# Attention heads on TensorE: the matmuls of a step put in another order

## Chip, cores and metric

One core of a Trainium2 chip runs the whole program. The metric is the time of one execution in microseconds (us). Engines are called as the profile calls them: PE is TensorE (PEld its weight loads), DVE is VectorE, ACT is ScalarE, POOL is GpSimd, SP is the queue that issues most DMAs.

## What is computed

Causal attention with a second term from a memory, for 4 x 8 = 32 heads of S = 576 rows and D = 64 columns, and behind it two MLP layers on 2304 tokens. The change touches the heads alone.

```python
scores = scale * q @ k.T                 # causal: -1e9 above the diagonal
a = exp(scores - scores.max(-1)); a /= a.sum(-1) + 1e-9
local = a @ v
q_p = where(q > 0, q, exp(q) - 1) + 1
mem_out = (q_p @ M_prev) / (q_p @ z_prev + 1e-6)
x = g * mem_out + (1 - g) * local        # g = sigmoid(beta) of the head
h = relu(x @ w_in); y = (s * h*h + b) @ w_out       # first MLP, d_ff 2048
# second MLP: softmax-gated unit, layer norm, product with the second w_out
```

## The kernel before

**Stages.** The program computes all heads, then the first MLP in five chunks of tokens, then the second MLP. In the profiled execution the regular part of the heads lies between about 50 and 226 us of the span, their end between 226 and 256 us, and the MLPs behind it.

**Two kinds of matmul.** Products of queries and keys are split in a high and a low part and run as fp32r; each is one matmul instruction. Everything else of a head is fp32: the product of weights and values and the memory product run as two instructions for each matmul call, and a transposition (a "turn") is one instruction. Each instruction has its own weight load in front of it.

**What PE does for head h.** `rows_of_scores(h, t)` (line 565) computes the scores of row tile t, only so that DVE can find the maximum of each row (`row_maximum`, line 967, written to `least`). The five tiles come in three groups: `first_rows` (tiles 4 and 1), `second_rows` (3), `third_rows` (0 and 2). All share two banks of PSUM, `ps_s`: tile 3 overwrites tile 4, and tiles 0 and 2 overwrite tile 1 and the turned maxima. So `second_rows` waits for DVE's maximum of tile 4, `third_rows` for that of tile 1 and for the copy of the turned maxima. The maxima of the head before are turned in the same group (line 594), copied by DVE (`negT`, line 976) and spread by POOL into `Q1` (line 394). Two steps later `cross(h, c)` (lines 631 and 632) computes the transposed scores of chunk c = 0 to 3, with the maxima already taken off by the second matmul of each block, into one of the two banks of `ps_x` (c mod 2); ACT takes the exponential (`exp_weights`, line 786, into `pT`), and POOL masks the diagonal tiles (line 406). One step after that `weigh_values(h, ts)` (line 650) multiplies `pT` with the values for the row tiles ts: tile t takes t + 1 calls, so two instructions times 1, 2, 3, 4, 5. The weights of tile 4 are 64 columns wide, those of the others 128, and so are those of one block of `cross(h, 0)` (64) and all other blocks (128).

**A step.** `steps` of `tensor` runs step h from 4 on: `first_rows(h+2)`, the crosses of head h, `weigh_values` of head h-1, `second_rows` and `third_rows` of head h+2, and work of pairs of heads. With pr = h // 2, an even step has `turn_output(pr-2)` and `turn_keys(pr+3)`, an odd step `turn_queries(pr+3)` and `memory(pr+1)`. A turn is five transpositions (line 486), memory is ten instructions (line 556). The last keys are turned in step 24, the last queries in step 25, the last rows of scores in step 29.

**What lies beside it.** Each engine works through its own program in order; semaphores are the only ties.
- DVE in step h: `first_rows` (copy of `negT`, two maxima), `second_rows`, `third_rows`; then in an even step `cut_keys(pr+3)` (line 1032, two instructions, after ACT's `round_keys`) and `scale_local(pr-1)` (lines 1057 to 1065), which divides the values product of a pair and frees the bank `ps_v` of the next pair's: `weigh_values` of an even head waits for it. In an odd step `scale_memory(pr+1)`.
- ACT: the four exponentials, and between them `copy_output`, `copy_queries`, `repeat_queries`, `feature_relu`, `feature_exp`, `round_keys` (line 818).
- POOL: masks, the spread of the maxima, rounding and cutting of the queries, `add_halves` (line 413), which makes the pair's output that `turn_output` turns; behind head 31 the cutting of the first MLP's weights (lines 1218 to 1229), for which PE's first MLP matmuls (line 1256) wait.
- SP: loads, and `stack`, which puts high and low halves one above the other after ACT's and POOL's cuts.

Of the kernel before, what the change touches and what calls it, by code (L numbers as in the profile page):

```python
# [12 lines left out]
P = 128  # L13
# [8 lines left out]
def need(eng, sem, value):  # L22

    if not isinstance(value, int) or value > 0:
        eng.wait_ge(sem, value)
# [84 lines left out]
def attention(nc, whole, ctx, xT, xq, ident, q, k, v, M_prev, z_prev, beta):  # L110
# [50 lines left out]
    least = [sb(f"least{s}", [P, P]) for s in range(2)]  # L161
# [50 lines left out]
    def is_pair(p):  # L212
        return 0 <= p < NPAIR

    def is_head(h):
        return 0 <= h < HEADS
# [264 lines left out]
    def tensor(pe):  # L481
# [24 lines left out]
        def turn_keys(p):  # L506
            pe.wait_ge(k_in[p % 2], 16 * Q_DMAS * (p // 2 + 1))
            if p == 0:
                pe.wait_ge(cleared_dve, PSUM_CLEARS)
            elif p == 1:  # L510
                act_placed(pe, 0, "k_own0")
                pe.wait_ge(k_lo_done, 1)
            else:
                pe.wait_ge(qT_copied, max(p, 3) if p != 3 else 4)
                need(pe, t_mem_done, p - 2)
                need(pe, xT_done, p - 4)
            turn(pair_tiles(first_k[p] if p < DIRECT else k_raw[p % 2]), kT_turned, keys_psum(p))
# [51 lines left out]
        def first_rows(h):  # L569
            if h == 0:  # L570
                pe.wait_ge(cleared, FOR_ROWS)
            if h < 2 * DIRECT:
                p = h // 2
                if h == 0:
                    act_placed(pe, 0, "q_hi1")
                    dve_placed(pe, 0, "q_lo0")
                elif h == 1:
                    act_placed(pe, 0, "q_hi1")
                    dve_placed(pe, 0, "q_lo1")
                elif h == 2:  # L580
                    act_placed(pe, 1, "q_cut0")
                    dve_placed(pe, 1, "q_lo0")
                else:
                    act_placed(pe, 1, "q_own1")
                    dve_placed(pe, 1, "q_lo1")
            elif h < HEADS:
                p = h // 2
                pe.wait_ge(stack_landed[p % SLOTS][h % 2], 16 * STACK_DMAS * stacks_sent(p))
            need(pe, maxed, 4 * min(h, HEADS))
            if h < HEADS:  # L590
                rows_of_scores(h, 4)
                ins = rows_of_scores(h, 1)
            if is_head(h - 1):
                ins = pe.transpose(ps_s[:, NEG_AT:NEG_AT + P], least[(h - 1) % 2][:, :], ident[:, :])
            ins.then_inc(scored, 1)

        def second_rows(h):
# [9 lines left out]
        def cross(h, c):  # L607
            a, p, par = slot(h), h // 2, h % 2
            kept = KEPT[par]
            if h == 0 and c == 0:  # L610
                pe.wait_ge(k_lo_done, 1)
                act_placed(pe, 1, "q_hi1")
                dve_placed(pe, 1, "q_lo0")
                pe.wait_ge(cleared, FOR_FIRST)
                pe.wait_ge(cleared_dve, DVE_CLEARS + 1)
            if h == 2 and c == 0:
                pe.wait_ge(cleared, POOL_CLEARS)
            if c == 0:
                pe.wait_ge(neg_spread, h + 1)
                if p < DIRECT:  # L620
                    pe.wait_ge(repeated, p + 1)
                    act_placed(pe, p, "q_own1")
                    pe.wait_ge(k_lo_done, p + 1)
                else:
                    pe.wait_ge(q_again, p - DIRECT + 1)
            need(pe, exped, h * NC + c - 1)
            at = 0
            for j, lo, hi in CHUNKS[c]:
                some = slice(P * j, P * j + rows_of[j])
                out = ps_x[0:rows_of[j], c % 2, at:at + hi - lo]  # L630
                pe.matmul(out, stacked[:, a, 1, some], stacked[:, a, 0, lo:hi], start=True, stop=False)  # L631
                ins = pe.matmul(out, K1[0:kept, p % LATE, par, some], Q1[0:kept, p % SLOTS, par, lo:hi],  # L632
                                start=False, stop=True)
                at += hi - lo
            ins.then_inc(crossed, 1)

        def weigh_values(h, ts):
            par = h % 2
            if 0 in ts:
                p = h // 2  # L640
                pe.wait_ge(tri_done, (h + 1) * NT)
                pe.wait_ge(v_in[p % 3], 16 * Q_DMAS * (p // 3 + 1))
                need(pe, t_loc_done, p)
                if h < 2:
                    act_placed(pe, 1, "k_own1")
                    pe.wait_ge(k_lo_done, 2)
            for t in ts:
                for j in range(t + 1):
                    at, m = p_at[j] + P * (t - j), rows_of[t]
                    ins = pe.matmul(ps_v[0:m, par, E1 * t:E1 * (t + 1)], pT[par][:, at:at + m],  # L650
                                    v_raw[h // 2 % 3][:, j, par, :], start=(t == 0),
                                    stop=(j == t), skip_group_check=True)
            if NT - 1 in ts:
                ins.then_inc(pv_done, 1)

        def steps(hs):
            for h in hs:
                pr, even = h // 2, h % 2 == 0
                ahead, here, behind = is_head(h + 2), is_head(h), is_head(h - 1)
                if ahead or is_head(h + 1):  # L660
                    first_rows(h + 2)
                if here:
                    cross(h, 0)
                if even and is_pair(pr - 2):
                    turn_output(pr - 2)
                if not even and is_pair(pr + 3):
                    turn_queries(pr + 3)
                if behind:
                    weigh_values(h - 1, (0, 1))
                if ahead:  # L670
                    second_rows(h + 2)
                if here:
                    cross(h, 1)
                if behind:
                    weigh_values(h - 1, (2,))
                if even and is_pair(pr + 3):
                    turn_keys(pr + 3)
                if ahead:
                    third_rows(h + 2)
                if here:  # L680
                    cross(h, 2)
                if behind:
                    weigh_values(h - 1, (3,))
                if here:
                    cross(h, 3)
                if not even and is_pair(pr + 1) and pr + 1 > 0:
                    memory(pr + 1)
                if behind:
                    weigh_values(h - 1, (4,))

        warm_up()
        turn_keys(0)
# [80 lines left out]
    def scalar(act):  # L773
# [8 lines left out]
        def exp_weights(h, c):  # L782
            act.wait_ge(crossed, h * NC + c + 1)
            if c == 0:
                need(act, pv_done, h - 1)
            act.activation(pT[h % 2][:, chunk_at[c]:chunk_at[c] + chunk_width[c]],  # L786
                           ps_x[:, c % 2, 0:chunk_width[c]], ACT.Exp, scale=SCALE).then_inc(exped, 1)
# [104 lines left out]
        def steps(hs, aside=None):  # L892
            for h in hs:
                pr, even = h // 2, h % 2 == 0
                here = is_head(h)
                if here:
                    exp_weights(h, 0)
                    if aside:
                        aside(0)
                if even and is_pair(pr - 2):  # L900
                    copy_output(pr - 2)
                if not even and is_pair(pr + 3):
                    copy_queries(pr + 3)
                if here:
                    exp_weights(h, 1)
                    if aside:
                        aside(1)
                if is_pair(pr + 2):
                    if even:
                        repeat_queries(pr + 2, 0)  # L910
                    else:
                        feature_relu(pr + 2)
                if even and is_pair(pr + 3):
                    round_keys(pr + 3)
                if here:
                    exp_weights(h, 2)
                    if aside:
                        aside(2)
                if is_pair(pr + 2):
                    if even:  # L920
                        repeat_queries(pr + 2, 1)
                    else:
                        feature_exp(pr + 2)
                if here:
                    exp_weights(h, 3)
                    if aside:
                        aside(3)

        def let_go():
            act.wait_ge(maxed, 4 * HEADS)  # L930
# [1219 lines left out]
```

## Time and profile before

| | |
|---|---|
| Median of 3 runs | 856.83 us (856.77 to 857.05) |
| The profiled execution's own time | 856.63 us |
| Its span in the profile | 854.5 us |
| PE busy | 842.5 us (99%) |
| DVE, ACT, POOL busy | 514.5, 340.6, 341.5 us (60%, 40%, 40%) |
| Granted TensorE clock | 9 in tenths in each of the 40 slices, 1.00 in the windows |
| Matmuls of the values, line 650 | 960, mean 254 ns |
| Rows of scores, line 565 | 192, mean 370 ns |
| Transposed scores, line 631 | 192, mean 320 ns |

How to read it: a matmul's record is longer than the time it takes of PE, because the next one starts before it has ended (960 matmuls of line 650 with a mean of 254 ns have 107.6 us of busy time between them). So what a matmul costs is read from the distance of starts, not from lengths. The record of a matmul and that of its weight load are two lines of the trace.

### The profile page before, as it was taken

The page shows a single profiled execution, that of the slowest core. Times are in us where ns is not written, and L with a number is a line of the kernel's source. Part 1 is how long each engine was busy: PE and PEld are TensorE (multiplying, and loading weights), DVE is VectorE, ACT ScalarE, POOL GpSimd, SP SyncE. Part 2 cuts the span into 40 slices and gives each one's busy share as a digit, 9 for nine tenths or more (in the row PEclk, how much of TensorE's full clock was granted, in tenths as well). Part 3 has the DMA queues.
Part 4 walks back from the last instruction along what each step waited for, and adds up shares of the span by engine and source line. Part 5 has one row for each costly group of instructions (what it writes and reads, how often), then busy time and mean ns, then how long its engine had stood idle before and what let it go on. Part 6 is the DMA issues. An engine that isn't in the chain of part 4 may idle for free.

```text
span 854.5 us, 13137 instructions
## 1 busy us (share of the span) xinstructions
PE 842.5 (99%) x4912; PEld 745.8 (87%) x4912; DVE 514.5 (60%) x1052; ACT 340.6 (40%) x607; POOL 341.5 (40%) x452
## 2 busy tenths in 40 slices
PE   8999999999999999999999999999999999999998
PEld 7899999999888888888888889999999888888886
DVE  7766657666547865433443334335767997777763
ACT  6665555565442223222322222224335534444422
POOL 5665656565659994000000000000648853334400
PEclk9999999999999999999999999999999999999999
DMA  8665666656403332000000000000101200000001
GB/s 147 141 150 131 149 144 135 149 129 132 119 5 106 107 105 75 1 0 1 1 1 0 1 1 1 1 1 1 30 21 49 62 26 25 26 25 17 21 25 49
DMA packets 86365, 49.35 MB, mean 58 GB/s; under 512 B 65056, under 2 KB 73248, under 8 KB 86304
## 3 DMA queue, kind: packets, MB, share of 16 engines
q1 hardware_dynamic: 83760, 47.94, 23.3%
q10 hardware_dynamic: 2544, 0.59, 0.4%
q8 instruction: 39, 0.64, 0.3%
q14 instruction: 22, 0.18, 0.1%
HBM read 27.28 MB, written 4.72 MB: 37 GB/s over the span
## 4 chain that ended last, share of the span: by engine, by line
PE 90%; DVE 7%; issue 2%; POOL 1%; ACT 0%; POOLq 0%; ACTq 0%
PE ps_h L1256 8%; PE ps_y L1273 8%; PE ps_h L1258 8%; PE ps_y L1272 8%; PE ps_h L1257 8%; PE ps_y L1271 8%; PE ps_v L650 7%; PE ps_s L565 4%; PE ps_r L1725 4%; PE ps_r L1724 4%; PE ps_r L1723 4%; PE ps_hid L1660 3%; PE ps_hid L1658 3%; PE ps_hid L1659 3%; DVE spent L967 3%
## 5 line engine op out<-in xcount | busy, mean ns | idle before, releaser
L1373 DVE TENSOR_TENSOR xT<-xT 128x512 f32<-128x512 f32 (+1 forms) x80 | 61.7, 772 | 125.6 <-ACT xT L1331 125.5
L1273 PE MATMUL ps_y<-g_hi,wout 128*128 128x512 f32 (+1 forms) x320 | 117.5, 367 | 0.0
L1272 PE MATMUL ps_y<-g_lo,wout 128*128 128x512 f32 (+1 forms) x320 | 117.5, 367 | 0.0
L1271 PE MATMUL ps_y<-g_hi,wout 128*128 128x512 f32 (+1 forms) x320 | 117.4, 367 | 0.0
L1557 POOL TENSOR_TENSOR win<-stage,win 128x512 fp32r<-128x512 f32 x2 | 2.6, 1294 | 281.8 <-ACT win L1792 281.8
L650 PE MATMUL ps_v<-v_raw,pT 128*128 128x65 f32 (+1 forms) x960 | 107.6, 254 | 1.2 <-DVE t_loc L1065 1.2
L650 PEld LDWEIGHTS ps_v<-v_raw,pT 128*128 128x128 f32 (+1 forms) x960 | 101.3, 173 | 6.9 <-issue 4.7
L967 DVE CUSTOM_DVE_ANT_0 spent<-ps_s,mask 128x576 f32<-128x576 f32 (+4 forms) x160 | 81.6, 539 | 42.4 <-PE ps_s L565 41.6
L1256 PE MATMUL ps_h<-x_hi,win 128*128 128x512 f32 (+1 forms) x280 | 103.0, 368 | 0.0
L1258 PE MATMUL ps_h<-x_hi,win 128*128 128x512 f32 (+1 forms) x280 | 102.8, 367 | 0.0
L1257 PE MATMUL ps_h<-x_lo,win 128*128 128x512 f32 (+1 forms) x280 | 102.8, 367 | 0.0
L1337 ACT ACTIVATE g_hi<-xT 128x512 fp32r<-128x512 f32 (+1 forms) x80 | 47.2, 590 | 137.2 <-DVE xT L1375 137.2
L786 ACT ACTIVATE pT<-ps_x 128x512 f32<-128x512 f32 (+3 forms) x128 | 64.2, 502 | 94.4 <-PE ps_x L632 93.5
L1331 ACT ACTIVATE xT<-ps_h 128x512 f32<-128x512 f32 (+1 forms) x80 | 44.2, 553 | 138.0 <-PE ps_h L1258 136.2
L1378 DVE TENSOR_TENSOR g_lo<-xT,g_hi 128x512 fp32r<-128x512 f32 (+1 forms) x80 | 65.8, 823 | 52.5 <-ACT g_hi L1337 52.5
L406 POOL TENSOR_SCALAR_AFFINE_SELECT pT<-pT 128x128 f32<-128x128 f32 (+1 forms) x160 | 42.7, 287 | 86.4 <-ACT pT L786 86.1
L1271 PEld LDWEIGHTS ps_y<-g_hi,wout 128*128 128x128 f32 x320 | 60.1, 188 | 7.6
L1273 PEld LDWEIGHTS ps_y<-g_hi,wout 128*128 128x128 f32 x320 | 60.1, 188 | 7.5
L1272 PEld LDWEIGHTS ps_y<-g_lo,wout 128*128 128x128 f32 x320 | 60.1, 188 | 7.4
L631 PE MATMUL ps_x<-stacked 128*128 128x448 f32 (+2 forms) x192 | 59.8, 320 | 0.6 <-POOL Q L394 0.4
L565 PE MATMUL ps_s<-stacked 128*128 128x512 f32 (+2 forms) x192 | 55.5, 370 | 4.2 <-DVE least L967 2.9
L1256 PEld LDWEIGHTS ps_h<-x_hi,win 128*128 128x128 f32 x280 | 52.5, 188 | 6.7
(211 smaller groups left out, 1804.9 us busy)
## 6 DMA issues: line engine op xcount, KB each, us to landing
stacked<-cut SPq DMA_DIRECT2D x56, 288.0 KB, 5.1
out<-res SPq DMA_DIRECT2D x18, 256.0 KB, 2.0
v_raw<-in_v SPq DMA_DIRECT2D x32, 128.0 KB, 3.3
stage<-in_moe_w_in SPq DMA_DIRECT2D x16, 256.0 KB, 2.8
stage<-in_moe_w_out SPq DMA_DIRECT2D x16, 256.0 KB, 2.6
k_raw<-in_k SPq DMA_DIRECT2D x28, 128.0 KB, 2.5
q_raw<-in_q SPq DMA_DIRECT2D x28, 128.0 KB, 3.6
stage<-in_moe_w_in SPq DMA_DIRECT2D x4, 512.0 KB, 3.6
```

Of the source, the lines that this page charges most:

```text
L565: ins = pe.matmul(ps_s[:, S_AT[t] + lo:S_AT[t] + hi], stacked[:, a, 0, P * t:P * (t + 1)], stacked[:, a, 1, lo:hi], start=True, stop=True)
L650: ins = pe.matmul(ps_v[0:m, par, E1 * t:E1 * (t + 1)], pT[par][:, at:at + m], v_raw[h // 2 % 3][:, j, par, :], start=(t == 0), stop=(j == ...
L786: act.activation(pT[h % 2][:, chunk_at[c]:chunk_at[c] + chunk_width[c]], ps_x[:, c % 2, 0:chunk_width[c]], ACT.Exp, scale=SCALE).then_inc( ...
L967: return dve.tensor_tensor_reduce(spent[:, at:at + n], ps_s[:, S_AT[t]:S_AT[t] + n], mask[:, FULL * P + r - n:FULL * P + r], -1.0, HUGE, A ...
L1256: pe.matmul(out, hi, x_hi[:, k, 0:n], start=(k == 0), stop=False)
L1257: pe.matmul(out, hi, x_lo[:, k, 0:n], start=False, stop=False)
L1258: ins = pe.matmul(out, lo, x_hi[:, k, 0:n], start=False, stop=(k == KT - 1))
L1271: pe.matmul(out, wout[:, f, HI, w], g_hi[:, r, 0:n], start=(f == 0), stop=False)
L1272: pe.matmul(out, wout[:, f, HI, w], g_lo[:, r, 0:n], start=False, stop=False)
L1273: ins = pe.matmul(out, wout[:, f, LO, w], g_hi[:, r, 0:n], start=False, stop=(f == FT - 1))
L1373: dve.tensor_tensor(r, r, r, ALU.mult).then_inc(square_done, 1)
L1378: dve.tensor_tensor(g_lo[:, f % RING, 0:width(c)], r, g_hi[:, f % RING, 0:width(c)], ALU.subtract)\
```

## The change

It reorders `steps` of `tensor`, changes `first_rows` there, and reorders `steps` of `scalar`. No instruction is added or removed, and none has another shape; no wait changes its value.

- In `first_rows` the maxima of the head before are turned ahead of the two row tiles and not behind them. The semaphore `scored` still counts up with the last matmul of the group.
- In a step of PE, `cross(h, 1)` comes directly behind `cross(h, 0)`; `weigh_values` is called for tiles 0, 1, 2 and for tiles 3, 4 in place of four calls; `second_rows` and `third_rows` stand together and directly ahead of `cross(h, 2)` and `cross(h, 3)`; `turn_keys` moves from between the values of tile 2 and `third_rows` to behind `cross(h, 3)`.
- ACT takes exponentials 0 and 1 together and 2 and 3 together; the copies that stood between them stand behind the first two, `round_keys` and `feature_exp` behind all four.
- The programs of DVE, POOL and SP are not touched, nor are the steps before step 4, which are written out one by one.

```diff
--- before.py
+++ after.py
@@ -587,11 +587,11 @@
                 p = h // 2
                 pe.wait_ge(stack_landed[p % SLOTS][h % 2], 16 * STACK_DMAS * stacks_sent(p))
             need(pe, maxed, 4 * min(h, HEADS))
+            if is_head(h - 1):
+                ins = pe.transpose(ps_s[:, NEG_AT:NEG_AT + P], least[(h - 1) % 2][:, :], ident[:, :])
             if h < HEADS:
                 rows_of_scores(h, 4)
                 ins = rows_of_scores(h, 1)
-            if is_head(h - 1):
-                ins = pe.transpose(ps_s[:, NEG_AT:NEG_AT + P], least[(h - 1) % 2][:, :], ident[:, :])
             ins.then_inc(scored, 1)
 
         def second_rows(h):
@@ -661,32 +661,25 @@
                     first_rows(h + 2)
                 if here:
                     cross(h, 0)
+                    cross(h, 1)
                 if even and is_pair(pr - 2):
                     turn_output(pr - 2)
                 if not even and is_pair(pr + 3):
                     turn_queries(pr + 3)
                 if behind:
-                    weigh_values(h - 1, (0, 1))
+                    weigh_values(h - 1, (0, 1, 2))
                 if ahead:
                     second_rows(h + 2)
-                if here:
-                    cross(h, 1)
-                if behind:
-                    weigh_values(h - 1, (2,))
-                if even and is_pair(pr + 3):
-                    turn_keys(pr + 3)
-                if ahead:
                     third_rows(h + 2)
                 if here:
                     cross(h, 2)
-                if behind:
-                    weigh_values(h - 1, (3,))
-                if here:
                     cross(h, 3)
+                if even and is_pair(pr + 3):
+                    turn_keys(pr + 3)
                 if not even and is_pair(pr + 1) and pr + 1 > 0:
                     memory(pr + 1)
                 if behind:
-                    weigh_values(h - 1, (4,))
+                    weigh_values(h - 1, (3, 4))
 
         warm_up()
         turn_keys(0)
@@ -897,34 +890,30 @@
                     exp_weights(h, 0)
                     if aside:
                         aside(0)
+                    exp_weights(h, 1)
+                    if aside:
+                        aside(1)
                 if even and is_pair(pr - 2):
                     copy_output(pr - 2)
                 if not even and is_pair(pr + 3):
                     copy_queries(pr + 3)
-                if here:
-                    exp_weights(h, 1)
-                    if aside:
-                        aside(1)
                 if is_pair(pr + 2):
                     if even:
                         repeat_queries(pr + 2, 0)
+                        repeat_queries(pr + 2, 1)
                     else:
                         feature_relu(pr + 2)
-                if even and is_pair(pr + 3):
-                    round_keys(pr + 3)
                 if here:
                     exp_weights(h, 2)
                     if aside:
                         aside(2)
-                if is_pair(pr + 2):
-                    if even:
-                        repeat_queries(pr + 2, 1)
-                    else:
-                        feature_exp(pr + 2)
-                if here:
                     exp_weights(h, 3)
                     if aside:
                         aside(3)
+                if even and is_pair(pr + 3):
+                    round_keys(pr + 3)
+                if not even and is_pair(pr + 2):
+                    feature_exp(pr + 2)
 
         def let_go():
             act.wait_ge(maxed, 4 * HEADS)
```

## Rows read from the trace of the kernel before

**Rows 1.** the page's section 1: busy us, share of the span, instructions

```profile
PE 842.5 (99%) x4912; PEld 745.8 (87%) x4912; DVE 514.5 (60%) x1052; ACT 340.6 (40%) x607; POOL 341.5 (40%) x452
```

**Rows 2.** windows view, head stage: stretch, busy us (count) by engine, granted clock, DMA

```profile
50.26:226.00 175.74, 174.63 (x1469) 163.28 (x1467) 112.50 (x359) 103.77 (x190) 108.62 (x192) 1.00 0.62 136
```

**Rows 3.** timeline of PE, odd step: start us, length us, engine, line, operation, count

```profile
191.16 0.78 PE L650 MATMUL ps_v<-v_raw,pT 128*128 128x65 f32 x6
192.02 0.50 PE L565 MATMUL ps_s<-stacked 128*128 128x512 f32 x1
192.35 0.25 PE L631 MATMUL ps_x<-stacked 128*128 128x192 f32 x1
...
196.46 0.80 PE L650 MATMUL ps_v<-v_raw,pT 128*64 128x65 f32 x10
```

**Rows 4.** timeline of PE, the even step behind it

```profile
197.19 0.72 PE L565 MATMUL ps_s<-stacked 128*128 128x512 f32 x3
...
198.97 0.78 PE L650 MATMUL ps_v<-v_raw,pT 128*128 128x65 f32 x6
...
199.87 0.25 PE L631 MATMUL ps_x<-stacked 128*128 128x192 f32 x1
...
203.12 0.31 PE L632 MATMUL ps_x<-Q,K 69*128 69x320 f32 x1
```

**Rows 5.** timeline of PE's weight loads, around the start of the even step

```profile
196.92 0.20 PEld L650 LDWEIGHTS ps_v<-v_raw,pT 128*64 128x64 f32 x2
197.18 0.53 PEld L565 LDWEIGHTS ps_s<-stacked 128*128 128x128 f32 x3
...
198.28 0.14 PEld L632 LDWEIGHTS ps_x<-Q,K 69*64 69x64 f32 x1
198.36 0.53 PEld L486 LDWEIGHTS ps_t<-ident,xq 128*128 128x128 f32 x5
198.86 0.75 PEld L650 LDWEIGHTS ps_v<-v_raw,pT 128*128 128x128 f32 x6
199.53 0.19 PEld L565 LDWEIGHTS ps_s<-stacked 128*128 128x128 f32 x1
199.64 0.19 PEld L631 LDWEIGHTS ps_x<-stacked 128*128 128x128 f32 x1
199.87 0.19 PEld L632 LDWEIGHTS ps_x<-Q,K 69*128 69x128 f32 x1
```

**Rows 6.** timeline of DVE, even step's end and odd step's start

```profile
188.02 0.08 DVE L967 DVE_READ_ACCUMULATOR2_ANT least<- 128x1 f32 x1
...
189.57 0.17 DVE L1057 SCALAR_TENSOR_TENSOR rl<-ps_v,inv_rest 128x10 f32<-128x10 f32 x1
...
190.88 0.29 DVE L976 COPY negT<-ps_s 5x128 f32<-5x128 f32 x1
191.20 0.76 DVE L967 CUSTOM_DVE_ANT_0 spent<-ps_s,mask 128x576 f32<-128x576 f32 x1
```

**Rows 7.** timeline of ACT, even step: the rounding of the keys, the last exponential

```profile
201.73 0.65 ACT L818 ACTIVATE cut<-ps_t 128x576 fp32r<-128x576 f32 x1
...
203.47 0.44 ACT L786 ACTIVATE pT<-ps_x 128x320 f32<-128x320 f32 x1
```

**Rows 8.** timeline of PE, last steps: [idle before <- releaser]

```profile
233.92 0.85 PE L650 MATMUL ps_v<-v_raw,pT 128*128 128x65 f32 x6 [0.20 <-DVE t_loc L1065]
...
235.28 0.25 PE L631 MATMUL ps_x<-stacked 128*128 128x192 f32 x1
...
247.26 0.85 PE L650 MATMUL ps_v<-v_raw,pT 128*128 128x65 f32 x6 [0.77 <-DVE t_loc L1065]
```

**Rows 9.** timeline of PE behind the last head

```profile
251.96 0.76 PE L486 MATMUL ps_t<-ident,xq 128*128 128x128 f32 x5 [0.47 <-POOL xq L413]
...
255.76 0.50 PE L1256 MATMUL ps_h<-x_hi,win 128*128 128x512 f32 x1
```

**Rows 10.** timeline of POOL, the first weights of the next stage

```profile
253.71 1.27 POOL L1221 TENSOR_TENSOR win<-stage,win 128x512 fp32r<-128x512 f32 x1
```

## The prediction

> **What bounds the kernel now.** I read the page's first section, then the windows by stage, then PE's timeline through one odd and one even step, then its weight loads there, and last the timelines of the engines that release it. The page says that PE is busy 99% of the span [rows 1]; in the regular part of the heads it is busy 174.63 of 175.74 us at a granted clock of 1.00 [rows 2]. So no other engine can be the bound for long, but "busy" hides two things that starts show.
>
> First, a wait. From the first matmul of the values to the first 192-column matmul of chunk 1 an odd step takes 192.35 - 191.16 = 1.19 us [rows 3], an even step with the same instructions 199.87 - 198.97 = 0.90 us [rows 4]. The odd one loses 0.29 us, ahead of the 512-column row tile at 192.02. What ended it is on DVE [rows 6]: behind the values of the pair DVE works 1.31 us on `scale_local` (189.57 to 190.88), then copies the turned maxima (0.29), then takes the maximum of tile 4 (0.76, to 191.96), and only then may tile 3 overwrite tile 4.
>
> Second, the price of a matmul. Weight loads start 0.11 us apart for 128 columns: the six of the values take 199.53 - 198.86 = 0.67 us [rows 5]. A load goes on while the matmul before it streams: the load of line 565 at 199.53 is followed by that of 631 at 199.64, and the next, behind the 512-column stream, at 199.87, that is 0.23 us later [rows 5]. So each instruction costs the larger of its own stream (0.23 for 512 columns) and the next load (0.11 for 128 columns, 0.06 for 64 columns), whatever type the neighbours have. The matmul records tell another story (the 512-column one begins at 199.55 and the next at 199.87, 0.32 us [rows 3, 4]), because the first of them is stamped while its own load still runs. The Trainium skill (Perfetto Trace Analysis, Per-instruction lifecycle, Tensor Engine) says that the start reported for a matmul is that of its data prefetch and its end an estimate; the loads here agree with that. Another rule there speaks otherwise (TensorE: Matmul & The Clock Gate, What overlaps and what doesn't: a weight load overlaps matmuls in flight only where the row groups differ). By it a 512-column instruction would cost 0.23 + 0.11 and no order would change PE's own time; the loads at 199.64 and 199.87 are 0.23 apart [rows 5], so the measurement decides against it.
>
> **The change on PE itself.** No instruction comes or goes, so only pairs of neighbours count. Every instruction followed by a 128-column load costs the same as before. Three junctions differ.
> - Transpositions load quickly: behind the 64-column block of chunk 0 the first load of a turn starts 0.08 us after the last one (198.28, 198.36), and the five of the turn take 198.86 - 198.36 = 0.50 us, of which the last four are 0.11 each, so the first is 0.06 [rows 5]. After the change a 192-column block with an ordinary load (0.11) stands there: 0.055 us more in each of the 25 steps 4 to 30 with a turn in that place (14 even, 11 odd), 1.4 us.
> - The keys' turn followed a load-bound values product, where its first load was cheaper by the same 0.055; now it follows a 320-column stream that hides any load: 11 x 0.055 = 0.6 us more.
> - The turned maxima (line 594) now follow the 64-column values, where a load stands bare: 0.06 in place of 0.11 for that load. I take 0.035 us gained (between 0.02 and 0.055) in 27 steps: 0.9 us less.
>
> Together +1.1 us. The gathering of types as such I cost at nothing, since the loads at the boundaries of [rows 5] (199.53 after 198.86) have the pitch of the others. One boundary is not shown before: fp32r weights of 64 columns followed by fp32r weights of 128. Its nearest rows are the turn behind the same block (0.08, so 0.02 over the plain 0.06) and the 64-column values followed by 128-column rows of scores: the two loads at 196.92 are 0.06 apart, and the next comes at 197.18, 0.20 after the second and so 0.09 more than a load's 0.11 [rows 5]. I take the first, because it is the same block; the second end would be 0.09 x 27 = 2.4 us more.
>
> **The wait of the odd step.** Both sides move, so I lay out an even step's end and the odd step after it. X is the start of the last 320-column matmul (203.12 [rows 4]).
> - PE: keys turned from X+0.15 to X+0.70; the values of tile 3, eight loads of 0.11, and of tile 4 (ten of 64 columns, 196.46 to 197.19 = 0.73 [rows 3, 4], plus 0.1 for the change of width) to X+2.4; maxima turned, first rows and chunk 0 (197.19 to about 198.37, 1.18 [rows 4, 5]) to X+3.6; chunk 1 with 0.06 + 0.11 + 0.11 + 0.13 + 0.13 to X+4.1; queries turned, 0.6, to X+4.7; twelve instructions of values, 1.3, to X+6.0, where tile 3 goes.
> - ACT: the last exponential from X+0.35, 0.44 long, to X+0.8 [rows 4, 7]; `round_keys` when the turn is written, X+0.95 to X+1.6 (0.65 [rows 7]). It is queued behind exponential 3 now; nobody but DVE waits for it.
> - DVE: `cut_keys` 1.52 from X+1.65 to X+3.15, `scale_local` 1.31 to X+4.45, maxima copied to X+4.8, tile 4 to X+5.6 [rows 6].
>
> So the values (X+4.7) find their bank free with 0.25 us to spare, and tile 3 (X+6.0) finds tile 4 read with 0.4. The cover ahead of tile 3 grows by chunk 1 and tile 2's values (0.5 + 0.7 us), and the delay of `cut_keys` takes some 0.9 of it back, since DVE used to reach `scale_local` right behind the values. Gone: 11 odd steps (5 to 25) x 0.29 = 3.1 us.
>
> Other waits: chunk 1 needs exponential 3 of the head before, which has the values of tiles 3 and 4 and the first rows for cover (over 2 us); chunks 2 and 3 need exponentials 0 and 1, with the turn and the values between (about 1.9 us for two exponentials, each about as long as the 0.65 of `round_keys` [rows 7]). ACT's and POOL's moved work has its users one or two steps later. SP's `stack` waits for the same things as before. I cost all of it at nothing; with the cover gone, an exponential would cost up to 0.65 us a head.
>
> **The end of the heads.** In steps 27 and 29 no queries are turned, so the values wait (0.20 idle at 233.92) and tile 3 again: 235.28 - 233.92 = 1.36 against 0.90, 0.46 lost [rows 4, 8]. No keys are cut in steps 26 and 28, so DVE is not late, and chunk 1 (0.5) and tile 2 (0.7) cover both: 2 x 0.66 = 1.3 us. In step 31 the values wait 0.77 [rows 8]; chunk 1 goes into that gap, 0.5 gained. The last but one output waits 0.47 for POOL's addition [rows 9], which stands behind the mask of exponential 1; that comes earlier: 0.45 gained. Behind the heads the first MLP matmul starts at 255.76, and its weights are ready at 253.71 + 1.27 = 254.98 [rows 9, 10]; POOL reaches them behind the last mask, which moves ahead of PE's end by about as much as PE waits less, so the gain passes on.
>
> **The sum.** 3.1 + 1.3 + 0.5 + 0.45 = 5.35 us gained, 1.1 paid: 4.3. The profiled execution's own time was 856.63 us, so 852.3; the median of the runs is 0.2 above it: **852.5 us**.
>
> **Rivals.**
> - A, the boundaries cost what the matmul records say: the first matmul behind another type begins 0.32 to 0.33 before its successor in place of 0.23 [rows 3, 4], and the last of the values is stamped 0.03 early. 0.08 x 3 boundaries fewer x 27 steps = 6.5 us more, and the 1.1 not paid: 845. Against it: the pitch of loads. 10%.
> - B, DVE becomes the bound of the odd step. `cut_keys` comes behind `round_keys` behind the moved turn. From `scale_local` starting after X+3.4 on, each 0.1 us is paid 11 times. If it is 0.8 late (an exponential or a copy of ACT ahead of `round_keys`), 0.55 x 11 = 6 us: 858.5, slower than before. Against it: ACT has nothing else ready by then. 9%.
> - C, the unshown boundary from 64 to 128 columns pays the upper price: +2.4, 854.9. 13%.
> - D, the wait stays at its old size though the cover grew, because the DVE chain moved with it: only the end gains, 3.1 less: 855.6. 8%.
> - E, nothing that can be told apart: the waits turn up elsewhere. 856.8. 4%.
>
> **Numbers.** The forecast has 56%; its own range is 851.0 to 854. The range of 8 in 10 takes in C, D and E and stops short of A and B: 847.5 to 856.8. A measurement of this kernel can tell about 0.2% (1.7 us) from no change, so faster means under 855.1: the forecast, A and two thirds of C, 0.75. Within: D, E and the rest of C, 0.16. Slower: 0.09.
>
> **What would show it.** Right: from the first values to tile 3 no idle time in odd steps, the idle times at 233.92 and 251.96 gone, the one at 247.26 about 0.3; even steps longer by under 0.1 us and odd ones shorter by 0.25; weight loads at boundaries 0.11 apart. A: both steps shorter by some 0.25 more, though no wait shows. B and D: waits of line 650 for line 1065 or of line 565 for line 967. C: a load 0.2 us behind the 64-column ones of chunk 0. I would be wrong above all if a moved copy of ACT or the late `cut_keys` held PE in each step.

## The result

The changed kernel takes 850.19 us (median of 4 runs, 849.83 to 850.93) against 856.94 us (4 runs, 856.77 to 857.37): a ratio of 0.9922, 95% interval 0.9904 to 0.9939, so 5.2 to 8.2 us less. Forecast were 852.5 us, 4.3 less. The sign and the wide range (847.5 to 856.8) held. The gain is more than half as large again as forecast, and 850.19 lies below the forecast's own range of 851.0 to 854. In a later run the same kernel took 850.62 us beside 857.33.

In the windows view of the changed kernel PE shows no idle time in the regular part of the heads, where [rows 2] had 1.1 us. Columns as there. Like the busy time, this view sees only what the matmul records leave open; small waits show in the starts alone.

```profile
50.04:221.30 171.26, 171.26 (x1468) 163.71 (x1466) 111.98 (x359) 103.75 (x190) 107.68 (x192) 1.00 0.63 138
```

The view of waits of PE over all heads has one line left, the wait in step 31:

```profile
PE ps_v L650 <- DVE t_loc L1054: 0.2, 1, 0.2
```

**An odd step and the start of the next.** PE's timeline; the first line answers to the turn ahead of [rows 3], the others to [rows 3, 4].

```profile
187.92 0.71 PE L486 MATMUL ps_t<-ident,q_raw 128*128 128x128 f32 x5
188.47 1.49 PE L650 MATMUL ps_v<-v_raw,pT 128*128 128x65 f32 x12
189.76 0.77 PE L565 MATMUL ps_s<-stacked 128*128 128x512 f32 x3
...
190.94 1.28 PE L556 MATMUL ps_t<-mz,fT 128*128 128x130 f32 x10
192.05 1.73 PE L650 MATMUL ps_v<-v_raw,pT 128*128 128x65 f32 x18
193.71 0.33 PE L591 MATMUL ps_s<-ident,least 128*128 128x128 f32 x1
```

From the first values to tile 3 there are 189.76 - 188.47 = 1.29 us for twelve instructions, where an even step takes 1.26 (195.96 to 197.22). The 0.03 is in the stamp of the first matmul and is no wait: by the loads, the kernel of experiment 5 has the same 1.34 us there (188.13 to 189.47) as this one (188.40 to 189.74). So the wait of 0.29 us in [rows 3] is gone. A small one stands elsewhere, ahead of the first values:

```profile
187.79 0.60 PEld L486 LDWEIGHTS ps_t<-ident,q_raw 128*128 128x128 f32 x5
188.40 1.41 PEld L650 LDWEIGHTS ps_v<-v_raw,pT 128*128 128x128 f32 x12
```

and in the kernel of experiment 5, where DVE is early:

```profile
187.57 0.60 PEld L486 LDWEIGHTS ps_t<-ident,q_raw 128*128 128x128 f32 x5
188.13 1.42 PEld L650 LDWEIGHTS ps_v<-v_raw,pT 128*128 128x128 f32 x12
```

From the queries' turn to the values it is 0.61 us here and 0.57 there (means of 11 odd steps): 0.04 us a step, and what they wait for follows.

**DVE and ACT in the same step**, the rows that answer to [rows 6, 7]. The first is ACT's `round_keys`, the second the two instructions of `cut_keys`:

```profile
184.77 0.65 ACT L811 ACTIVATE cut<-ps_t 128x576 fp32r<-128x576 f32 x1
```

```profile
185.45 1.52 DVE L1021 TENSOR_TENSOR K<-ps_t,cut 64x576 fp32r<-64x576 f32 x2 [0.70 <-ACT cut L811]
187.01 0.17 DVE L1046 SCALAR_TENSOR_TENSOR rl<-ps_v,inv_rest 128x10 f32<-128x10 f32 x1
187.21 0.22 DVE L1051 RECIPROCAL rl<-rl 128x10 f32<-128x10 f32 x1
187.46 0.82 DVE L1054 TENSOR_TENSOR t_loc<-ps_v,rl 128x640 f32<-128x640 f32 x1
188.32 0.29 DVE L965 COPY negT<-ps_s 5x128 f32<-5x128 f32 x1
```

With the last 320-column matmul at 183.87 as X, the timetable of the prediction is read against the trace: `round_keys` X+0.90 (forecast X+0.95), `cut_keys` X+1.58 (X+1.65), bank free at 188.28 = X+4.41 (X+4.45), values X+4.60 (X+4.7). DVE now idles 0.70 us for the late keys, and its chain ends 0.12 us ahead of the first load of the values (188.28, 188.40). In all 11 odd steps this distance is 0.115 to 0.117 us, the same as in experiment 4, where PE clearly waits for DVE; in experiment 5 it is over 0.3. So the values start as soon as the bank is free, which is the 0.04. Tile 4 has been read at X+5.53 (forecast X+5.6), 0.34 us ahead of the load of tile 3. In [rows 6] the first line is a read of 0.08 us where the two instructions of `cut_keys` were meant; this is the line of the kernel before that the prediction's 1.52 us stands on:

```profile
188.02 1.52 DVE L1032 TENSOR_TENSOR K<-ps_t,cut 64x576 fp32r<-64x576 f32 x2
```

**Weight loads** of the changed kernel, answering to [rows 5]:

```profile
193.50 0.14 PEld L650 LDWEIGHTS ps_v<-v_raw,pT 128*64 128x64 f32 x1
193.71 0.14 PEld L591 LDWEIGHTS ps_s<-ident,least 128*128 128x128 f32 x1
193.71 0.58 PEld L565 LDWEIGHTS ps_s<-stacked 128*128 128x128 f32 x3
...
194.75 0.14 PEld L632 LDWEIGHTS ps_x<-Q,K 69*64 69x64 f32 x1
194.81 0.19 PEld L631 LDWEIGHTS ps_x<-stacked 128*128 128x128 f32 x1
194.93 0.19 PEld L632 LDWEIGHTS ps_x<-Q,K 69*128 69x128 f32 x1
...
198.26 0.61 PEld L486 LDWEIGHTS ps_t<-ident,k_raw 128*128 128x128 f32 x5
198.84 1.70 PEld L650 LDWEIGHTS ps_v<-v_raw,pT 128*128 128x128 f32 x18
```

Behind the 64-column block of chunk 0 the next load comes 0.06 us later (194.75, 194.81) and the one after it 0.12: the boundary from 64 to 128 columns within fp32r is free, so rival C is out. The turn of the keys takes 0.58 us of loads (198.26 to 198.84). Behind the last load of the 64-column values (193.50) the next one comes after 0.21 us, as in [rows 5] (the second load of the pair at 196.92, then 197.18).

**Where the time went.** A step is measured from the 64-column piece of its first rows to that of the next (means of 11 regular steps of each kind; us):

| | before | after | less | forecast less |
|---|---|---|---|---|
| odd steps 5 to 25, each | 7.791 | 7.473 | 11 x 0.318 = 3.50 | 2.97 |
| even steps 4 to 24, each | 6.902 | 6.895 | 11 x 0.007 = 0.08 | -0.83 |
| steps 26 and 28 | 6.400, 6.400 | 6.338, 6.343 | 0.12 | -0.04 |
| step 27 | 7.713 | 6.889 | 0.82 | 0.70 |
| step 29's start to the first MLP matmul | 23.04 | 20.91 | 2.13 | 1.59 |
| start of step 4 | 50.59 | 50.44 | 0.15 | 0 |

Together 6.8 us, the difference of the spans (854.5 and 847.7). The last column is worked out from the prediction's unrounded terms and adds up to 4.4. The start of step 4 lies between 50.4 and 51.1 us in the thirteen profiles of this case, whatever the kernel, so up to 0.7 us between two profiles is start-up; in the two kernels that were profiled twice the mean steps repeat within 0.003. Where the start-up could blur a verdict, the steps decide.

### The profile page after: what moved, and what is told of

Read it like the earlier page. It is cut to its first block, busy times and chain, and to the rows that moved or that the text cites. A ratio compares the mean times of both kernels' runs of the same rounds, so it can differ in the third digit from the quotient of the medians.

```text
span 847.7 us, 13137 instructions
## 1 busy us (share of the span) xinstructions
PE 838.3 (99%) x4912; PEld 745.8 (88%) x4912; DVE 512.6 (60%) x1052; ACT 340.0 (40%) x607; POOL 340.4 (40%) x452
## 4 chain that ended last, share of the span: by engine, by line
PE 96%; DVE 2%; ACT 1%; ACTq 1%; issue 0%; POOL 0%; POOLq 0%
PE ps_v L650 10%; PE ps_h L1245 8%; PE ps_y L1260 8%; PE ps_h L1247 8%; PE ps_y L1262 8%; PE ps_y L1261 8%; PE ps_h L1246 8%; PE ps_r L1714 4%; PE ps_r L1712 4%; PE ps_r L1713 4%; PE ps_s L565 4%; PE ps_hid L1649 3%; PE ps_hid L1647 3%; PE ps_hid L1648 3%; PE ps_x L631 3%; PE ps_t L486 3%
## 5 line engine op out<-in xcount | busy, mean ns | idle before, releaser
L650 PE MATMUL ps_v<-v_raw,pT 128*128 128x65 f32 (+1 forms) x960 | 102.9, 256 | 0.3 <-DVE t_loc L1054 0.2
L956 DVE CUSTOM_DVE_ANT_0 spent<-ps_s,mask 128x576 f32<-128x576 f32 (+4 forms) x160 | 79.5, 538 | 36.7 <-PE ps_s L565 35.9
L650 PEld LDWEIGHTS ps_v<-v_raw,pT 128*128 128x128 f32 (+1 forms) x960 | 98.0, 173 | 3.5 <-issue 0.9
L779 ACT ACTIVATE pT<-ps_x 128x512 f32<-128x512 f32 (+3 forms) x128 | 60.9, 504 | 88.0 <-PE ps_x L632 87.9
L1245 PEld LDWEIGHTS ps_h<-x_hi,win 128*128 128x128 f32 x280 | 52.6, 188 | 6.6
L1247 PEld LDWEIGHTS ps_h<-x_hi,win 128*128 128x128 f32 x280 | 52.5, 188 | 6.6
L1246 PEld LDWEIGHTS ps_h<-x_lo,win 128*128 128x128 f32 x280 | 52.6, 188 | 6.6
```

Source lines behind the costliest of these rows:

```text
L956: return dve.tensor_tensor_reduce(spent[:, at:at + n], ps_s[:, S_AT[t]:S_AT[t] + n], mask[:, FULL * P + r - n:FULL * P + r], -1.0, HUGE, A ...
L1245: pe.matmul(out, hi, x_hi[:, k, 0:n], start=(k == 0), stop=False)
L1246: pe.matmul(out, hi, x_lo[:, k, 0:n], start=False, stop=False)
L1247: ins = pe.matmul(out, lo, x_hi[:, k, 0:n], start=False, stop=(k == KT - 1))
```

## The experiments

Each run is compared with the kernel before on the same chip. Changes that are parts of the change, or that move one thing in it, tell the terms apart. A boundary pair is one way from fp32r instructions to fp32 ones and one back. This table has all of them (medians in us, steps as above):

| | median | before there | even step | odd step |
|---|---|---|---|---|
| maxima first | 856.10 | 857.04 | 6.859 | 7.785 |
| values 3 and 4 together | 855.79 | 857.04 | 6.853 | 7.787 |
| chunk 1 ahead | 852.69 | 857.04 | 6.947 | 7.538 |
| changed, two boundary pairs more | 855.07 | 857.04 | 6.892 | 7.917 |
| changed, keys early | 849.57 | 856.86 | 6.841 | 7.433 |
| keys early, two boundary pairs more | 849.20 | 856.86 | 6.830 | 7.437 |
| changed, values 4 ahead of 3 | 851.39 | 856.86 | 6.944 | 7.492 |
| keys early, chunks 0 and 1 exchanged | 848.00 | 856.86 | 6.807 | 7.413 |
| changed, ACT's old order | 850.36 | 857.33 | 6.894 | 7.471 |
| changed, again | 850.62 | 857.33 | 6.895 | 7.470 |
| chunks exchanged, again | 848.12 | 857.33 | 6.807 | 7.412 |

**1. The maxima first, alone.**

```diff
+            if is_head(h - 1):
+                ins = pe.transpose(ps_s[:, NEG_AT:NEG_AT + P], least[(h - 1) % 2][:, :], ident[:, :])
             if h < HEADS:
                 rows_of_scores(h, 4)
                 ins = rows_of_scores(h, 1)
-            if is_head(h - 1):
-                ins = pe.transpose(ps_s[:, NEG_AT:NEG_AT + P], least[(h - 1) % 2][:, :], ident[:, :])
```

> The kernel before with one part of the change: the turned maxima ahead of the two row tiles in the first rows. Theory (what counts on TensorE is the pitch of weight loads: an instruction costs the larger of its own stream and the next load; behind the 64-column values a load stands bare): the bare load is that of a transposition, 0.06 in place of 0.11 us, and the pair of gaps around the old place (0.131 and 0.097 in the trace) closes up: 0.05 us less in each even step, 1.3 us less in all, 855.6, with the wait of the odd steps taking part of it back (it ends on DVE, whose semaphore comes no earlier), so 856.0 is as likely. Rival A (a boundary between fp32r and fp32 costs 0.08 us by itself): one boundary pair fewer in 27 steps, 2.2 us less, 854.7; even steps shorter by 0.08 to 0.15.

Ratio 0.9989 (0.998 to 0.9998). Even steps are 0.043 shorter, odd ones the same, since there the wait for DVE takes it back. The term is 0.043 and not 0.035, and about half of the least that rival A asks for (0.08).

**2. The values of tiles 3 and 4 together, alone.**

```diff
                     cross(h, 2)
-                if behind:
-                    weigh_values(h - 1, (3,))
-                if here:
                     cross(h, 3)
                 ...
-                    weigh_values(h - 1, (4,))
+                    weigh_values(h - 1, (3, 4))
```

> The kernel before with one part: the values of tile 3 moved from between crosses 2 and 3 to directly ahead of those of tile 4, crosses 2 and 3 together. Theory: the 64-column values are entered from a values instruction with a stream of 0.057 us where they were entered from a 320-column stream (0.148) or from memory (0.11), and the load of the first 64-column weights is bare whatever stands before it; so 0.055 us less in each step with values (27), 1.5 us less: even steps 6.85 in place of 6.90; the DVE-ended wait of the odd steps is as long or longer, as it starts behind the last values. 855.4. Rival A: the same plus one boundary pair fewer, 0.08 x 27 more: 853.2 and even steps 6.77.

Ratio 0.9988 (0.9979 to 0.9997). Even steps are 0.049 shorter, odd ones again held by the wait. This is the term that the prediction lacked. It is less than the 0.13 of rival A (6.90 to 6.77).

**3. Chunk 1 directly behind chunk 0, alone** (TensorE and the exponential).

```diff
                     cross(h, 0)
+                    cross(h, 1)
                 ...
-                if here:
-                    cross(h, 1)
```

> The kernel before with one part: chunk 1 of the crosses directly behind chunk 0 on TensorE, and exponential 1 directly behind exponential 0 on ScalarE. The number of boundaries between types stays as it was. Theory: the 0.49 us of chunk 1 now lie ahead of the values and of tile 3, so the odd step's wait of 0.28 us for DVE goes (11 x 0.28 = 3.1 us), those of steps 27 and 29 shrink by 0.5 each, steps 31 and 32 gain 0.9 together; the turns lose their cheap first load (0.055 less the 0.02 of the old junction, 25 times: 0.8 us). 856.8 - 4.2 = 852.6; odd steps 7.54, even steps 6.94. Rival A: nothing but the waits in this part, and it explains less than half of the 6.7 us of the whole change: 853.5 or above.

Ratio 0.9958 (0.9946 to 0.9971), 4.35 us less. Even steps are 0.045 longer, the price of the turn's first load that is no longer cheap; odd steps are 0.253 shorter net, so 0.30 without that price, all of the wait. This part alone brings two thirds of the whole; with the 0.94 and 1.25 us of the first two the parts add up to 6.5.

**4. Two boundary pairs more in the changed kernel.** `weigh_values` takes a range of calls, and two of tile 3's four stand around `cross(h, 2)`.

```diff
                     third_rows(h + 2)
+                if behind:
+                    weigh_values(h - 1, (3,), (0,))
                 if here:
                     cross(h, 2)
+                if behind:
+                    weigh_values(h - 1, (3,), (1,))
+                if here:
                     cross(h, 3)
                 ...
-                    weigh_values(h - 1, (3, 4))
+                    weigh_values(h - 1, (3,), (2, 3))
+                    weigh_values(h - 1, (4,))
```

> The changed kernel with two more boundary pairs in each step and nothing else: the first matmul call of the values of tile 3 stands between third rows and cross 2, the second between crosses 2 and 3. All junctions made so are between 128-column weights. Theory: 0.00 us by the pitch of the loads, at most 0.01 a step: 850.2 within 0.3, steps of 7.47 and 6.90 as in the changed kernel. Rival A (a boundary pair costs 0.08 us): 2 x 0.08 x 27 = 4.3 us more, 854.5, steps longer by 0.16.

The time came out at 855.07, which is what rival A said, and for another reason. Even steps are as in the changed kernel (6.892 against 6.895): the boundaries cost nothing. Odd steps are 0.44 longer. DVE's timeline there, and PE's:

```profile
189.84 1.52 DVE L1027 TENSOR_TENSOR K<-ps_t,cut 64x576 fp32r<-64x576 f32 x2 [1.15 <-ACT cut L817]
191.40 0.17 DVE L1052 SCALAR_TENSOR_TENSOR rl<-ps_v,inv_rest 128x10 f32<-128x10 f32 x1
191.60 0.22 DVE L1057 RECIPROCAL rl<-rl 128x10 f32<-128x10 f32 x1
191.85 0.82 DVE L1060 TENSOR_TENSOR t_loc<-ps_v,rl 128x640 f32<-128x640 f32 x1
```

```profile
192.83 1.52 PE L650 MATMUL ps_v<-v_raw,pT 128*128 128x65 f32 x12 [0.24 <-DVE t_loc L1060]
```

The four instructions moved ahead of the keys' turn hold the keys back by 0.45 us and shorten what PE does behind them by the same, so DVE frees the bank (192.67) 0.4 us too late. This is rival B's mechanism, started by 0.45 us: the changed kernel has nothing to spare there. The weight loads show the same wait under another name:

```profile
192.80 1.42 PEld L650 LDWEIGHTS ps_v<-v_raw,pT 128*128 128x128 f32 x12 [0.46 <-POOL pT L406]
```

That mask is of head h, whose values come a step later, and not of head h-1; in the changed kernel the two masks of that place run from 188.22 to 188.70 and the load starts at 188.40, so the values do not wait for them. The distance from DVE's end to the load is what stays, 0.12 us in both.

**5 and 6. The keys turned early**, between the values of tile 2 and the second rows, and rounded ahead of exponential 2; then the same two boundary pairs in that kernel.

```diff
                 if behind:
                     weigh_values(h - 1, (0, 1, 2))
+                if even and is_pair(pr + 3):
+                    turn_keys(pr + 3)
                 if ahead:
                     second_rows(h + 2)
                     third_rows(h + 2)
                 if here:
                     cross(h, 2)
                     cross(h, 3)
-                if even and is_pair(pr + 3):
-                    turn_keys(pr + 3)
```

> The changed kernel, but the keys are turned between the values of tile 2 and the second rows, and ScalarE rounds them ahead of exponential 2; everything else as in the changed kernel. Theory: in the odd steps of the changed kernel VectorE's chain (cut of the keys, scaling of the values, maxima) is just late (a wait of 0.04 us is left), and moving the split values into it cost 0.44 us a step; with the keys 1.2 us earlier the chain is off the path: odd steps 7.43 in place of 7.47. The first load of the keys' turn is cheap again: even steps 6.86 in place of 6.90. 11 x 0.08 = 0.9 us less than the changed kernel: 849.3. Rival (the chain does not matter here): only the load, 849.8.

> The run before with the keys turned early, and in it the two extra boundary pairs: the first two matmul calls of the values of tile 3 stand ahead of and behind cross 2. Theory (boundaries between fp32r and fp32 cost nothing, and what the split cost in the changed kernel was VectorE's chain being held back by the later turn of the keys): the same time as with the keys early and no split, 849.3 within 0.3, even and odd steps the same within 0.01. Rival A: 0.08 x 2 x 27 = 4.3 us more. Rival that the split itself makes a wait whatever the place of the keys: odd steps stay at 7.9, 854.

Keys early: even steps 0.054 and odd ones 0.040 shorter than in the changed kernel, as forecast from both terms (849.57, ratio 0.9914). With two boundary pairs more, 849.20 and the same steps within 0.011. DVE and PE of that kernel:

```profile
184.26 1.52 DVE L1027 TENSOR_TENSOR K<-ps_t,cut 64x576 fp32r<-64x576 f32 x2
...
186.27 0.82 DVE L1060 TENSOR_TENSOR t_loc<-ps_v,rl 128x640 f32<-128x640 f32 x1
```

```profile
187.51 1.45 PE L650 MATMUL ps_v<-v_raw,pT 128*128 128x65 f32 x12
```

DVE no longer waits for ACT, the bank is free at 187.09 and the values come 0.42 us later. So the 0.44 us of experiment 4 were the chain and nothing else, and a boundary between fp32r and fp32 at 128 columns has no price that shows (0.011 us a step at most, and that a gain).

**7. Values of tile 4 ahead of tile 3** (`(4, 3)` for `(3, 4)`).

> The changed kernel with the values of tile 4 ahead of those of tile 3. The same instructions and the same boundaries between types. Theory of the loads: leaving the 64-column weights, the bare load is one of 128 columns of values (0.11) in place of the turned maxima's (0.06), and entering them costs as before: 0.055 us a step, 27 steps, 1.5 us more than the changed kernel: 851.7, even steps 6.95. Rival A, which knows only types: no change, 850.2.

851.39 us, even steps 0.049 longer; odd ones only 0.019, because the 0.04 of wait that is left there gives way (0.57 us from the queries' turn to the values again). Types and boundaries are the same. The size came out as expected, but the expectation left out a part: by the starts of the single loads, the way into the 64-column values costs 0.31 us behind the keys' turn or memory, in place of 0.26 behind the values of tile 3, and the two loads that follow the first one on the way out are 0.05 later in all. Against these two stands the load of the turned maxima, which now follows 128-column values after 0.06 us, 0.05 sooner than a 128-column load would. So the run confirms that the neighbours of the 64-column values set the price and does not part the way in from the way out.

**8. Chunks 0 and 1 exchanged, keys early.** `CHUNKS` and `DIAG_AFTER` swap their first two entries, `chunk_at` keeps the places in `pT`, and one small clear of PSUM is added at the start.

> The kernel with the keys early, and chunks 0 and 1 of the crosses exchanged (tiles 3 and 0 first, then 1 and 4), so that the turn of queries or output follows the 64-column block again, whose load pitch is short; ScalarE's and GpSimd's orders of chunks follow, and one small clear of PSUM is added at the start. Theory: 0.046 us less in each of the 25 steps with such a turn (what chunk 1 ahead of the turn cost when it was moved alone), 1.1 us less: 848.2, even steps 6.82, odd steps 7.39. Rival: the 0.046 had another cause (the junction from 64 to 128 columns within fp32r), then no change: 849.3.

848.00 us (0.9897, 0.9883 to 0.9911) and 848.12 on another chip, the best of all. Weight loads of an even step there:

```profile
194.34 0.14 PEld L632 LDWEIGHTS ps_x<-Q,K 69*64 69x64 f32 x1
194.42 0.53 PEld L486 LDWEIGHTS ps_t<-ident,xq 128*128 128x128 f32 x5
194.91 1.42 PEld L650 LDWEIGHTS ps_v<-v_raw,pT 128*128 128x128 f32 x12
```

The turn behind the 64-column block takes 0.49 us of loads, against 0.57 for the same turn in the kernel of experiment 5, where it follows a 288-column stream. Of 0.046 forecast per step 0.034 (even) and 0.020 (odd) came. By the starts of the single loads, the last 64-column load and the first of the turn save 0.05 together in an even step, and the crosses ahead of them take 0.015 more in their new order; why they do, and why another 0.01 goes in an odd step between the turn and the rows of scores, is open.

**9 to 11. ACT's old order, the changed kernel again, the exchange again.**

> The changed kernel with ScalarE's order of the kernel before; TensorE as changed. Exponential 1 then stands behind the copy of the turned queries or output, and the rounding of the keys ahead of exponentials 2 and 3, which are held by it for about 1 us. Theory: each exponential has 1 us or more of other TensorE work between its product and its first user, and the rounding starts when the keys are turned in either order: no change, 850.2 within 0.4, steps 7.47 and 6.90. Rival (ScalarE's order carries part of the gain): TensorE waits at chunk 1 or 3 for exponentials, 0.1 to 0.6 us a step, 853 to 860.

> The changed kernel once more, beside the two others of this call on one chip: 850.2 within 0.4; steps of 7.47 and 6.90 us. It tells how much the start of the program (which differed by up to 0.6 us between profiles) adds to comparisons made across chips.

> The kernel with the keys early and chunks 0 and 1 exchanged once more, on the same chip as the changed kernel: 848.0 to 848.4, 2 us less than the changed kernel: steps of 7.41 and 6.81, 11 x (0.06 + 0.09) = 1.7 us from the regular steps and a few tenths from the end.

ACT's old order gives 850.36 and the same steps within 0.002: with TensorE's new order, ACT's part of the diff brings nothing that can be measured. On one chip the exchange is 2.5 us faster than the changed kernel (848.12, 850.62).

## Why the prediction was right or wrong

- **The bound and the odd step's wait: right.** The wait for DVE behind `scale_local` was there, and its going is the largest part: 0.29 forecast, 0.30 by experiment 3. The timetable's times for `round_keys`, `cut_keys`, the bank and the reading of tile 4 held within 0.07 us. Its spare time did not. Without a wait the first load of the values would start at X+4.49, 0.2 us before the forecast X+4.7 and 0.08 behind the bank's release, and the prediction put nothing for the 0.12 us that pass from DVE's end to the load. So the old wait is gone whole and a new one of 0.04 us has begun ahead of the values, 0.4 us in 11 steps, and experiment 4 showed that each further delay is paid in full.
- **A matmul costs the larger of its stream and the next load, whatever the types: right, except on the way into and out of the 64-column values**, where about 0.09 us come on top (last section). What rival A would have read off the matmul records is shown wrong by experiments 4 and 6: two boundary pairs more in every step, and steps equal within 0.011 where DVE's chain does not interfere. The Trainium skill's rule that a weight load overlaps matmuls in flight only where the row groups differ (TensorE: Matmul & The Clock Gate, What overlaps and what doesn't) finds no support in any run here: with a load of full height between them, 512-column rows of full height and what follows stay 0.23 us apart ([rows 5]: 199.64, 199.87).
- **"Three junctions differ": wrong, there are four, and this is the step that failed.** The prediction priced every instruction ahead of a 128-column load as before and left out that tile 3's last values instruction now stands ahead of the 64-column weights. In the traces these weights are not loaded under the stream before them, so an instruction in that place costs its own stream (about 0.06 us for one of the values, an estimate from the distance of the 64-column loads) and no longer a load of 0.11. The loads show it: from the last load ahead to the first of the 64-column values it was 0.385 us in the even steps and 0.313 in the odd ones, and it is 0.260 in both now (lines below the list). In an even step most of the difference is the 320-column stream, which has to be paid elsewhere; net it is 0.049 in experiment 2, in 28 steps: 1.4 us of the 2.4 that were missed. The prediction had the row for it (`x10` of 64 columns in [rows 3]) and used it only as a lump of 0.73 plus 0.1.
- **The other prices** were small and each a little off, all to the same side: the turn's first load 0.045 for 0.055, the maxima 0.043 for 0.035, the keys' place 0.040 (what the whole change has more than its three parts in an even step) to 0.054 (experiment 5) for 0.055. In 25, 27 and 11 steps: 0.25, 0.2 and up to 0.15 us.
- **The end of the heads:** forecast 0.70 + 1.59 us net for steps 27 and 29 to 32, measured 0.82 + 2.13, so 0.66 more. About 0.2 of it is the missing term in four steps. Another 0.24 I had not priced at all: in step 30 the output's turn started 0.30 us behind the last 64-column matmul (240.73 and 241.03 in the trace before, 0.06 in an undisturbed step), and that gap is gone too. The other 0.2 is not assigned. The gap of [rows 8] in step 31 was to fall from 0.77 to about 0.3: the trace has 0.2 idle (241.45), and the 0.47 of [rows 9] is gone, as forecast. The first MLP weights are ready at 246.91 + 1.27 = 248.18, before PE's first MLP matmul at 248.96, so the gain passed on.
- **Rivals B and D:** B's mechanism is real: the change as made runs into it by 0.04 us in each odd step, and every further delay would be paid. D is out by experiment 3.

The way into the 64-column values in an even step, before the change and after it; the second load of the pair at 199.51 starts at 199.62.

```profile
202.98 0.19 PEld L632 LDWEIGHTS ps_x<-Q,K 69*128 69x128 f32 x1
203.36 0.25 PEld L650 LDWEIGHTS ps_v<-v_raw,pT 128*64 128x64 f32 x3 [0.19 <-issue]
```

```profile
199.51 0.30 PEld L650 LDWEIGHTS ps_v<-v_raw,pT 128*128 128x128 f32 x2
199.88 0.13 PEld L650 LDWEIGHTS ps_v<-v_raw,pT 128*64 128x64 f32 x1
```

## What to carry to other kernels

Where TensorE is busy all the time, price a new order pair by pair, as the larger of an instruction's stream and the next weight load, and go through all pairs that are new, those inside a lump too. Then lay out the other engines' chain against it with its spare time: most of this gain was one wait of 0.3 us in every second step, and two orders that TensorE's own cost could not tell apart (850.2 and 855.1) were 5 us apart by that chain. A result that agrees with a rival in its total (855.07 for 854.5) may still refute it step by step.

## What was not expected of the hardware

The fp32 weights of 64 columns (tile 4's values) behave unlike all others here. Between their last load and the next load of another kind 0.21 us pass (193.50, 193.71), against 0.06 behind fp32r weights of 64 columns (194.75, 194.81). Of the 0.21 one such load and one such stream explain 0.12, so about 0.09 is neither. The way in has the same rest, worked out from the starts of single loads: 0.385 us behind two 320-column streams of 0.148, 0.313 behind memory instructions of 0.112, 0.308 behind transpositions of 0.109 (experiment 7), and 0.260 behind the values, 0.112 and 0.058; each time 0.09 is left over. It is paid twice in each head by every kernel of this case. No run tells whether it is the width, the type or the 64 rows of output that brings it.

When the pause on the way out ends, the load of a transposition and the load behind it start together (both 193.71) and the next follows 0.17 us later, which is 0.06 + 0.11 as for any others: only the load in the middle is stamped early. Why the exchanged chunks gave 0.01 to 0.03 us a step less than they should is open in part (experiment 8).
